# A recurrent attention scan with two feed-forward blocks: feed-forward products moved between the scan's steps, and products of the identity in its first rounds

## The reference

```python
for t in range(S):                                    # attention
    cur = einsum('bhd,bhe->bhde', u * k[t], v[t])
    y[t] = einsum('bhd,bhde->bhe', r[t], state + cur)
    state = w[t][:, :, :, None] * state + einsum('bhd,bhe->bhde', k[t], v[t])
x = tokens(y)                                         # (B, S, 384)
xn = (x - mean) / sqrt(var + 1e-6) * g_ln             # first block, 384 -> 1536 -> 384
x = x + maximum(xn @ w_ch1, 0) @ w_ch2
h = maximum(x @ w_in, 0); u, v = halves(h)            # second block, 384 -> 2 x 512
v_n = (v - mean(v)) / sqrt(var(v) + 1e-6)
v_s = einsum('ts,bsd->btd', w_spatial, v_n) + b_spatial
out = (u * v_s) @ w_out
```

## Time and profile before

| | |
|---|---|
| median of 3 runs | 541.44 us (541.2 to 541.72) |
| profiled execution | 542.48 us, its span 540.7 us |
| TensorE busy | 465.5 us, 86% |
| VectorE / ScalarE / GpSimd busy | 214.4 / 151.1 / 128.7 us |
| granted TensorE clock as the profile gives it | 1.00 in every slice |
| TensorE waits for VectorE's selections (L808) | 46.9 us in 35 waits |
| first products of the rounds start at | 8.29, 19.22, 36.40, 55.05, 77.20, 104.50, 125.29, 142.95, 160.75, 179.21, 198.19, 216.59, 235.12 us |

### The profile page before, as it was taken

How to read it: one execution, slowest core, us unless ns; L and a number is a source line. 1 busy time by engine, 2 the same in 40 slices (tenths; PEclk the granted TensorE clock), 3 DMA queues, 4 the chain that set the end, 5 groups by cost and what they waited for, 6 DMA issues and landing times.

```text
span 540.7 us, 11776 instructions
## 1 busy us (share of the span) xinstructions
PE 465.5 (86%) x4988; PEld 444.5 (82%) x4988; DVE 214.4 (40%) x492; ACT 151.1 (28%) x326; POOL 128.7 (24%) x148
## 2 busy tenths in 40 slices
PE   2587784768777787799999999999999999999997
PEld 2477673757676787689999999999999999898997
DVE  1554535164445534522145224322423267431130
ACT  3033233141233133223232123222222174311112
POOL 2445435153456345444200000000001052000000
PEclk9999999999999999999999999999999999999999
DMA  7431231212312311012000000000032010000102
GB/s 212 125 102 40 68 104 38 68 32 73 103 50 58 104 46 45 4 30 64 26 1 0 1 0 2 2 0 1 0 96 81 0 51 9 0 15 31 45 0 89
DMA packets 26553, 24.57 MB, mean 45 GB/s; under 512 B 1666, under 2 KB 23426, under 8 KB 26500
## 3 DMA queue, kind: packets, MB, share of 16 engines
q1 hardware_dynamic: 26500, 23.80, 14.8%
HBM read 21.44 MB, written 2.36 MB: 44 GB/s over the span
## 4 chain that ended last, share of the span: by engine, by line
PE 80%; DVE 8%; issue 8%; ACT 1%; POOL 1%; DMA 1%; DVEq 0%; SPq 0%; POOLq 0%; ACTq 0%
PE bank L1147 11%; PE bank L1148 10%; PE bank L1149 10%; PE low_bank L1049 8%; PE bank L1094 6%; DVE near L808 4%; PE high_bank L1149 4%; PE high_bank L1148 4%; PE high_bank L1147 4%; PE high_bank L1049 4%; PE low_bank L1147 3%; PE low_bank L1149 3%; PE low_bank L1148 3%; PE bank L1092 3%; PE low_bank L1028 2%
## 5 line engine op out<-in xcount | busy, mean ns | idle before, releaser
L1049 PE MATMUL low_bank<-rin,kin 64*64 64x32 f32 x1536 | 51.4, 291 | 48.1 <-DVE near L808 46.9
L1049 PEld LDWEIGHTS low_bank<-rin,kin 64*64 64x64 f32 x1536 | 47.2, 219 | 53.4 <-issue 50.6
L501 POOL TENSOR_TENSOR kin<-kin,wtot 128x256 f32<-128x256 f32 x60 | 52.2, 877 | 62.2 <-PE low_bank L1049 56.1
L518 POOL TENSOR_TENSOR vrstd<-vmv,half 128x1 f32<-128x1 f32 x12 | 7.7, 644 | 156.5 <-DVE vmv L979 156.5
L1094 PE MATMUL bank<-vin,score 128*128 128x48 f32 x192 | 44.6, 386 | 0.0
L1094 PEld LDWEIGHTS bank<-vin,score 128*128 128x128 f32 x192 | 44.2, 321 | 0.0
L769 DVE TENSOR_TENSOR rin<-rin,wtot 128x256 f32<-128x256 f32 x60 | 27.4, 457 | 34.7 <-PE low_bank L1049 18.7
L598 ACT COPY score<-near 64x512 f32<-64x512 f32 x24 | 14.8, 618 | 91.5 <-DVE near L808 91.3
L499 POOL TENSOR_TENSOR kin<-kin,win 128x256 f32<-128x256 f32 x12 | 12.4, 1031 | 74.7 <-PE low_bank L1049 74.7
L896 DVE SCALAR_TENSOR_TENSOR h11l<-bank,h11h 128x384 fp32r<-128x384 f32 x24 | 13.4, 558 | 38.5 <-ACT h11h L663 38.5
L511 POOL TENSOR_TENSOR ffw<-stage,ffw 128x384 fp32r<-128x384 f32 (+1 forms) x25 | 27.5, 1100 | 2.4 <-ACT ffw L584 2.4
(11 more groups left out here) (203 smaller groups left out, 1188.1 us busy)
## 6 DMA issues: line engine op xcount, KB each, us to landing
stage<-in_w SPq DMA_DIRECT2D x12, 384.0 KB, 3.3
kin<-in_kT SPq DMA_DIRECT2D x12, 256.0 KB, 4.4
rin<-in_rT SPq DMA_DIRECT2D x12, 256.0 KB, 4.3
win<-in_wT SPq DMA_DIRECT2D x12, 256.0 KB, 4.3
vin<-in_v SPq DMA_DIRECT2D x12, 192.0 KB, 3.4
out<-ob SPq DMA_DIRECT2D x12, 192.0 KB, 1.9
stage<-in_w_in SPq DMA_DIRECT2D x4, 384.0 KB, 3.2
x<-in_w_sp SPq DMA_DIRECT2D x4, 384.0 KB, 4.4
```

The source lines that it names most:

```text
L501: last = gp.tensor_tensor(k, k, wr[:, :, :, None].to_broadcast([P, NPR, m, c]), ALU.mult)
L1049: mm = te.matmul(dst[s0:s0 + Q, NPR * e + a, 0:Q // 2], kin[i % 4][lo:hi, a, s0:s0 + Q], r[:, :, 1, :], start=True, stop=True)
```

## The change

Every engine's program of the scan is rewritten over one numbering of the 52 slots, k = 4 s + j. From slot 20 (round 5) on, each slot k holds `F1(k-20)` and `F2(k-21)`, so 32 of the 48 F1 and 31 of the F2 are formed between the scan's steps; the V, U and X2T steps are placed anew among the 16 pairs that are left. To make room in PSUM, from tile 4 on the high levels are written beside the low ones (`upper_bank`), with waits on each other's selections, and during the slots F1 has a single bank (`f1_bank`), so that it waits for `h1_lo` of the pair before it. In slots 0 to 19 TensorE forms five products of the identity with itself in every slot (`keep_going`), whose result nobody reads. The products of `attend` are split into two halves of 64 output rows. `XT` of tiles 0 to 10 all stand in the scan. In rounds 1 to 4 VectorE selects a low level before it scales r for the high one. Loads and weight chunks get slots of their own (`weight_slots`).

```diff
+ALONE = 4
+N_KEEP = 5
-        b_f1 = [b_first, b_second]
-        b_acc = [low_bank[:, 0, :], low_bank[:, 1, :], high_bank[:, 0, :]]
-        b_vu = [high_bank[:, 1, :], b_y]
+        b_f1 = [b_first, low_bank[:, 0, :]]
+        b_acc = [high_bank[:, 0, :], high_bank[:, 1, :], b_third]
+        b_vu = [low_bank[:, 1, :], b_y]
+        def upper_bank(i, n):
+            o, c = (0 if i < ALONE else Q // 2 if n < N_MASKED else Q), min(LEVELS[n], Q)
+            return (high if i < ALONE else low)[:, :, o:o + (Q // 2 if n < N_MASKED else c)]
+        def f1_bank(n):
+            return b_f1[n % 2 if n >= N_BESIDE else 0]
...
+        N_SLOTS = N_LOW * (NT + 1)
+        SLOT_F1 = N_LOW * (ALONE + 1)
+        N_BESIDE = N_SLOTS - SLOT_F1
+        def f1_of(k):
+            return k - SLOT_F1 if k >= SLOT_F1 else None
+        def weight_slots(n):
+            if n < W1C // STAGE:
+                return [1 + 3 * n, 2 + 3 * n]
+            m = n - W1C // STAGE
+            return [SLOT_F1 - 1 + 2 * m, SLOT_F1 + 2 * m]
...
 SyncE
+            for k, s, j in slots_of_scan():
+                if j == 0 and 4 <= s + 2 < NT:
+                    load_w(s + 2)
+                    load_k(s + 2)
+                    load_r(s + 2)
+                if j == 1 and 3 <= s + 1 < NT:
+                    load_v(s + 1)
+                for n, part in weight_parts(k):
+                    if part == 1:
+                        load_chunk(n + 2)
...
 ScalarE
+                if f1_of(k) is not None:
+                    h1_hi(f1_of(k))
...
 VectorE
+            for k, s, j in slots_of_scan():
+                if s < NT:
+                    r_right(s, j)
+                if s > ALONE and j < N_HIGH:
+                    r_right(s - 1, N_LOW + j)
+                if j == 0 and s < NT:
+                    own_select(s)
+                if s < NT:
+                    select(s, j)
+                if 1 <= s <= ALONE and j < N_HIGH:
+                    r_right(s - 1, N_LOW + j)
+                if j < N_MIDDLE and s >= 1:
+                    select(s - 1, N_LOW + j)
+                for i, n in decay_plan(s, j):
+                    decays(i, n)
...
+                if j == 3 and s >= 2:
+                    turned_lo(s - 2, "XT", (s - 2) // TG, (s - 2) % TG)
+                n = f1_of(k)
+                if n is not None:
+                    h1_lo(n)
+                    if n and n % NF == 0:
+                        add_f2(n // NF - 1)
...
@@ TensorE @@
                     for e in range(2):
-                        mm = te.matmul(b_y[:, at + e * HD:at + (e + 1) * HD], score[:, NPR * e + a, :],
-                                       vin[i % 3][:, 2 * a + e, :], start=first(i), stop=first(i) or e == 1)
+                        for lo, hi in HALF:
+                            mm = te.matmul(b_y[lo:hi, at + e * HD:at + (e + 1) * HD], score[:, NPR * e + a, lo:hi],
+                                           vin[i % 3][:, 2 * a + e, :], start=first(i), stop=first(i) or e == 1)
...
+                if n and n <= N_BESIDE:
+                    te.wait_ge(h1_lo_ready, n)
...
+            def keep_going(k):
+                if k == 0:
+                    te.wait_ge(consts_loaded, 48)
+                for _ in range(N_KEEP):
+                    te.matmul(b_third[:, 0:P], idt[:, :], idt[:, :], start=True, stop=True)
+            for k, s, j in slots_of_scan():
...
+                if j == 3 and s >= 1:
+                    attend(s - 1)
+                n = f1_of(k)
+                if n is None:
+                    keep_going(k)
+                if n is not None:
+                    first_product(n // NF, n % NF)
+                    if n:
+                        second_product((n - 1) // NF, (n - 1) % NF)
+                if j == 0 and s >= 2 and carries(s - 2):
+                    gain(s - 2)
+                if j == 2 and s >= 2:
+                    turn(s - 2, "XT", (s - 2) // TG, (s - 2) % TG)
+                if j == 3 and s >= 1 and carries(s - 1):
+                    turn_k(s - 1)
```

More of the change, by code:

```diff
@@ L451, in _ @@
             sp.dma_start(idt[:, :], ident).then_inc(consts_loaded, 16)
[L452 to L457, removed]
+            for i in range(1, 4):
                 load_w(i)
@@ L525, in _ @@
             gp.memset(half[:, :], -0.5)
[L526 to L536, removed]
+            for k, s, j in slots_of_scan():
+                if s < NT:
+                    k_left(s, j)
+                if s >= 1 and j < N_HIGH:
+                    k_left(s - 1, N_LOW + j)
+                if s >= 2 and j == 1:
+                    inv_std(mv, rstd, s - 2, x_var_ready, x_rstd_ready)
+                for n, part in weight_parts(k):
+                    weight_lo(n, part)
             inv_std(mv, rstd, NT - 1, x_var_ready, x_rstd_ready)
@@ L632, in split_vn @@
                 sc.copy(vns[b][0][:, c * DH:(c + 1) * DH], vn[:, i, :]).then_inc(vn_hi_ready, 1)
[L634 to L658, removed]
             def h1_hi(n):
@@ L915, in decay_plan @@
                 return []
-            decays(0, 0)
[L918 to L935, removed]
-                            decay_state(s - 2)
-                    if j == 1 and s >= 2 and carries(s - 2):
-                        next_state(s - 2)
-                    if j == 2 and s >= 2:
-                        for part in range(3):
-                            x_stats(s - 2, part)
-                    if j == 3 and 3 <= s < 3 + TG:
-                        turned_lo(s - 3, "XT", 0, s - 3)
@@ L944, in _, with add_f2 @@
-            for n in range(EARLY):
-                h1_lo(n)
+            def add_f2(g):
+                dve.wait_ge(f2_done, NF * (g + 1))
+                for tt in range(TG):
+                    i = TG * g + tt
+                    ve.tensor_tensor(x[:, i, :], b_acc[tt][:, 0:D], x[:, i, :], ALU.add).then_inc(x2_ready, 1)
+            decays(0, 0)
+            for k, s, j in slots_of_scan():
+                if s < NT:
[4 more added lines that the diff above has]
+                    own_select(s)
+                if s < NT:
+                    select(s, j)
[5 more added lines that the diff above has]
+                    decays(i, n)
+                if j == 0 and s >= 2:
+                    for part in range(3):
+                        x_stats(s - 2, part)
+                    if carries(s - 2) and not first(s - 2):
+                        decay_state(s - 2)
+                if j == 1 and s >= 2:
+                    if carries(s - 2):
+                        next_state(s - 2)
+                    norm(s - 2)
+                if j == 3 and s >= 2:
+                    turned_lo(s - 2, "XT", (s - 2) // TG, (s - 2) % TG)
[4 more added lines that the diff above has]
+                        add_f2(n // NF - 1)
@@ L1170, in _, with second_product @@
-            tr, vu = TG, 0
+            def second_product(g, f):
+                n = NF * g + f
+                te.wait_ge(h1_hi_ready, n + 1)
+                te.wait_ge(h1_lo_ready, n + 1)
+                if f == 0 and g:
+                    te.wait_ge(x2_ready, TG * g)
+                if n == 0:
+                    te.wait_ge(blocks_placed, ALONE)
+                if g == 0:
+                    split_waits(te, (W1C + f * D) // STAGE)
+                w = slice(f * D, (f + 1) * D)
+                for tt in range(TG):
+                    sl = slice(tt * P, (tt + 1) * P)
+                    mm = split_product(b_acc[tt][:, 0:D], h1[n % 2][0][:, sl], h1[n % 2][1][:, sl],
+                                       w2s[0][:, w], w2s[1][:, w], f == 0, f == NF - 1)
+                mm.then_inc(f2_done, 1)
```

212 lines of the change are left out of this document (109 added, 103 removed).

## The result

The changed kernel takes 453.16 us (median of 4 runs, 453.11 to 455.56) against 541.58 us before; the ratio is 0.8378, with a 95% interval of 0.835 to 0.8406. The forecast was 459 us. The profiled execution has a span of 451.3 us.

What follows compares the result with a forecast made beforehand. The scan was taken as a TensorE-VectorE chain at the lower clock, the rest as a full TensorE. 8.3 (start) + 76.5 + 179 + 194 = 457.8, plus 1.8 outside the span, 459.6, stated as 459 us; 8-in-10 range 438 to 496.

Steps and rivals of the forecast that it cites:

- early rounds: Scan rounds 0 to 4, given identity products in 20 slots: 76.5 us at the upper clock level against 96.2 before.
- late rounds: Scan rounds 5 to 12, each slot now holding F1 and F2: 23.4 us a full round, 179 us together.
- dense stage: The part after the scan, where TensorE is full: loses 63 product groups, from 300.0 to 194 us.
- The reading of the clock: Whole scan: product spacing, not the clock column, shows TensorE at 1.2 GHz; the change can fill waits and raise the clock.
- small products unchanged: Scan's 64x32 products in the late rounds: no faster at the upper clock level, 6.50 us a round.
- rival D: Scan's small products follow the clock too, 3.2 us less in each of eight rounds: 433 us; chance 0.05.
- All waits are covered: Late rounds: TensorE has 5.1 us of work in a slot against a 3.32 us chain, covering all 3.65 us of waits.
- The stall: Near slot 11, where the decays of tile 4 wait for w(5): between nothing and 8.9 us, taken as 5.5.
- My two ends for them: Ten records of a slot's five identity products in rounds 0 to 4: 2.28 us at the lower clock level, 1.14 upper.
- Rival A: Rounds 0 to 4: the clock stays low, 106 us instead of 76.5, total 489 us; chance 0.12.
- C: Late rounds: the clock falls in every slot, up to 603 us, near 520 if in half the rounds; chance 0.06.
- B: Slots of the late rounds: a wait on `h1_lo` or the selections, 1 us in each of 32: 491 us; chance 0.07.

## Why the prediction was right

| term | predicted | measured |
|---|---|---|
| start | 8.3 | 7.9 |
| early rounds | 76.5 | 79.6 |
| late rounds | 179 | 166.9 |
| dense stage | 194 | 197.0 |

**The reading of the clock.** That the scan ran at the lower level although the column said 1.00 was right, and much of the forecast rests on it: 30 us of the kernel before come back by products that compute nothing (the identity products in it). A reader who takes the 1.00 at its word prices what is left of the scan by its records there, whole `attend` at 5.12 us where the upper level takes 2.6.

**Dense stage.** 194 against 197.0. The 3 us are waits that I had costed at nothing: TensorE waits 2.0 and 0.7 us at two transposes of `x`, once for VectorE's `xnT1l` and once for its addition to x. Three groups' V and U beside 16 pairs are not quite free.

**Late rounds.** The sum failed at one size: small products unchanged. I took 6.50 us of them in a round and put the halved price at 5% as rival D. They fell to 0.52 for the own term and 1.03 for a pair of levels, so 0.9 + 1.81 of the first slot became 1.55. Over round 10 the small products take 3.81 us, 2.69 less than I took. The round was priced at 23.4 and took 20.85, 2.55 less; `attend`, `turn_k` and `XT` cost 0.5 us more than priced and the changes between product sizes 0.4 less. That is rival D's mechanism: halved, the small products would have given 3.2. (The prediction gives their worth as 35 us in one place and, in rival D, as 26; eight rounds at 2.7 are some 20.) My argument, that 64 columns cost what 32 do and so columns and clock do not matter, took one for the other: a level went from 0.82 to 0.49 us with the clock, 51 to 31 ns a product and 26 to 15 ns a record, of which a plain float32 product has two. I had also held the floor of 25 ns in the Trainium skill ("TensorE: Matmul & The Clock Gate", section "Wait — 56ns, not 53.3ns?") against these products and concluded that they gain nothing. The trace does not bear this out: by record 15 ns lies below that floor, by product 31 ns above it, and which of the two it counts no run here shows. Either way my step from it was wrong.

**What gave it back.** Rounds 5 and 6 took 23.91 and 21.66 instead of 20.8. They hold waits of 0.76, 1.23, 0.99, 0.22 and 1.00 us, and the second fall of the clock. Round 12 took 17.7 (from 236.65) where 16.5 was forecast. "All waits are covered" was right for rounds 8 to 11 and wrong where GpSimd stands behind ScalarE; I had read the order of GpSimd's work, but not which part raises the semaphore.

**Early rounds.** 11.5, 13.5 and 15.3 were forecast for rounds 0, 1 and 4, and 11.07, 13.04 and 14.47 came. The stall was taken at 5.5 and was 6.47, in the place named. What was missing is what it does to the clock: 11.5 us at the lower level, in which the identity products cost 2.43 us a slot (56.23 to 58.66) instead of 1.3. My two ends for them (2.28 and 1.14) were right to 15%. That they raise the clock was right for the kernel before; in this one they hold it and yet are worth only 1.5 us, since without them the early rounds take 80.95 us. Rival A priced something else at 30 us, identity products that run at the lower level all through, and that came only behind the stall.

**`attend` in halves.** Predicted 1.4 us, measured 1.73; whole it takes 2.6. Its worth in the changed kernel is 9.6 us (462.75 against 453.16).

**The total.** That 459 came within 6 us is in part luck: the small products made the late rounds some 20 us shorter than the sum had them, waits, the fall of the clock and round 12 gave back about 8, and the early rounds and the dense stage 3 us each.

**Rivals.** C had 6%. Even without the other two parts the clock fell only once in the late rounds, for 6.8 us, and not in every slot. Its price took 4.6 us of products as what a rise needs; that was one observation, and in the changed kernel TensorE worked 11.5 us at the lower level behind the stall and 3.4 us behind the second fall. B did not come: the waits on `h1_lo` are 2.0 us in all.

## What to carry to other kernels

Judge TensorE's clock by the spacing of one and the same product at two places before sizing anything; here a TensorE that looked 77% busy ran the whole scan at the lower level, and filling its waits with real work paid twice, by the waits and by faster products. Filler products are worth something only while nothing better does the same: 30 us in the kernel before (240 of them), 9 beside the moved products (100 of them), 1.5 once `attend` ran in halves too, none after the stalls were gone. When one engine splits a chunk in parts for another, look at which part raises the semaphore, and at what stands behind the one that waits.

## What the runs showed of the hardware that I had not expected

The granted clock of the profile reads 1.00 up to the first recorded change, even where the chip is at 1.2 GHz: in the kernel before it reads 1.00 in all slices, the stretch from 241.15 to 245.31 with products 0.320 us apart among them, and in the kernel with the moving alone 1.00 from 97 to 110 us with the same spacing at 99. Two other executions of the kernel before give a mean of 0.813 and 0.851 over the span at 541.43 and 540.28 us, the same time. Once it has fallen in a trace it reads 0.50 and agrees with the spacing.

Small products of 64x64 weights and 32 columns follow the clock, but not in full: 0.82 us to 0.49 for 16 of them.

A product with 64 output rows, alternating between the halves, takes well under half of one over 128 rows: `attend` goes from 2.6 to 1.73 us at the upper level and from 5.12 to 3.16 at the lower, although it has twice the products. In the kernel before, the clock rises in most rounds once `attend` is in halves, where with whole ones it stayed at the lower level through the whole scan. The cause of that is open.

Behind one wait of 6.5 us TensorE worked 11.5 us at half clock. What exactly made the clock fall at 95.0, after waits of 0.76 and 1.23 us, was not settled: with whole `attend` the same two places have waits of 0.73 and 1.22 us (ended at 98.29 and 100.64), and the clock reads 1.00 through that round.
